# The start of a fused attention and two-layer-pair kernel: another order of its first 24 slots, and low halves of g1 on GpSimd

## The chip, the cores and the metric

The kernel runs on one core of a Trainium2 chip. The core has TensorE (PE in the profile; PEld is its loading of weights), VectorE (DVE), ScalarE (ACT), GpSimd (POOL) and SyncE (SP), which here issues the DMAs. The metric is the device time of one execution in microseconds (us), the median of several runs.

## The reference, cut to what matters

```python
scores = (q @ k.T) / sqrt(64)              # B 4, H 8, S 576, D 64
scores = where((rel >= 0) & (rel < 128), scores - slope[h] * rel, -1e9)
x = softmax(scores) @ v                    # to (2304, 512)
h = x @ w_in                               # 512 -> 2048
P = a0 + a1*h + a2*h**2 + a3*h**3
Q = 1 + |b0|*|h| + |b1|*h**2
y = (P / (Q + 1e-6)) @ w_out               # 2048 -> 512
h = y @ w2_in                              # 512 -> 2048
out = where(h > 0, h, exp(min(h, 0)) - 1) @ w2_out
```

## The kernel before

All products with weights are made of three products in fp16: each operand is scaled by a power of two and split into a high and a low half. The weights are w0 to w3 (`moe_w_in`, `moe_w_out`, and the two of the second pair). A weight comes in eight pieces of 512 KB. Before it can be split, its scale must be known. For this `gram` multiplies each piece with itself into one bank (a "norm product", 8 products of 128x128 each), `column_norms` takes the largest of each row, `top_turn`, `top_across` and `top_over` bring the largest of all to every partition, and `top_scales` makes the scale. The same is done for v, whose first three pieces (n = 0 in `TOPS`) serve the first tiles and whose other nine the later ones. Then ScalarE makes the high half of a piece (`piece_high`) and VectorE the low half (`piece_low`). `TOP_AT`, `GRAM_AT` and `SPLIT_AT` are the slots in which this happens.

The program is one loop over slots s from `FIRST` = -10, written out for every engine in its own order; semaphores join the engines. In slot s:

- Attention works on unit u = s + 10, one pair of heads of one block of 128 queries. TensorE makes the scores (`qk`), VectorE adds the distances (`bias_scores`), ScalarE takes the exponent, VectorE the reciprocals, GpSimd or (from slot 0 to 13) ScalarE normalises, TensorE turns the probabilities (`turn`), ScalarE copies them (`copy_probs`), TensorE multiplies them with v (`pv`), and ScalarE and VectorE write the halves of x (`split_x`, `low_x`). Every fourth slot the next block's queries and keys are turned and copied. In slots -10 to -7 the scores are 128 wide, in slots -6 to -1 they are 256 wide.
- From slot 0 on there is one step of the first pair per slot: `up1` (24 products of 256 columns) for 256 hidden columns of 256 tokens, then `evac1` on ScalarE, `denominator` and `polynomial` on VectorE, `log_exp` on ScalarE, `rational` on VectorE. In the next slot come `high1` on ScalarE and `low1` on VectorE, the two halves of g1, and `down1` takes them two slots after `up1`. Scales and bounds that these steps need come from `factors1(0)` for the first two tiles and `factors1(1)` for the later ones, 17 instructions of VectorE each on numbers of one column, in slots -2 and 7.
- From slot 14 (`LATE`) on there is the second pair too (`up2`, `elu`, `low2`, `down2`). 

SyncE issues the DMAs in a fixed order: queries, keys and v for block 0, v's first pieces, w0 with block 1 in between, then by slot the pieces of w1, the other nine pieces of v, and w2 and w3 as their places come free. The scores go to `score`, one buffer of two halves. Of PSUM's banks `ps_a` and `ps_b` take the scores, `ps_u1` and `ps_u2` the hidden products in turn, and `ps_u2` the norms of w2 and w3. Because of the latter, `up1` stands behind the scores in slots that follow a slot with a norm (3, 5 and 9).

## Time and profile before

| what | value |
|---|---|
| median of 3 runs | 990.9 us (990.37 to 993.07) |
| profiled execution, its own time | 992.75 us |
| profiled execution, span from first to last instruction | 991.0 us |
| TensorE, VectorE, ScalarE, GpSimd busy | 94%, 66%, 61%, 6% of the span |
| bytes moved | 46.72 MB |

A row of a timeline has the start and the length of an instruction, its engine, its line, and what it writes and reads; in brackets stands how long the engine sat idle before it, and what released it. Instructions of one engine can overlap a little; its pace is read from starts. Line L1070 is the bias of the scores, L1168 the denominator, L1107 the low half of a piece, L870 its high half, L509 a norm product, L1196 the low half of g1.

### The profile page before, as it was taken

Reading aid. Unit: us, or ns where it says so; the run is one execution under the profiler, and the core shown is the slowest. Engines: PE = TensorE matmul, PEld = TensorE weight load, DVE = VectorE, ACT = ScalarE, POOL = GpSimd, SP = SyncE. Lnnn points to the kernel's source line nnn. Section 1 sums busy time; section 2 is a strip of 40 time slices with the busy share of each in tenths; the row PEclk is TensorE's granted clock in tenths of the full one; section 3 lists DMA queues with packets and bytes.
Section 4 is the critical chain, followed back from the end, with each engine's and each line's share of the span. In section 5 each row is a group of like instructions: output and inputs, shape, how many; then the busy total and the mean of one; then the engine's idle time right before and its main releaser. Section 6 shows DMA issues by size and latency. Waiting matters only on the chain.

```text
span 991.0 us, 19531 instructions
## 1 busy us (share of the span) xinstructions
PE 934.5 (94%) x7692; PEld 715.1 (72%) x7692; DVE 654.3 (66%) x1430; ACT 601.6 (61%) x1189; POOL 55.4 (6%) x62
## 2 busy tenths in 40 slices
PE   6768889799999999999999999999999999999896
PEld 4557767577777777777777777777777777877563
DVE  4767878988876667666766676666766766663232
ACT  2767768877666666666666666666565655563332
POOL 1200000000000000000000000000000000000000
PEclk9878999899999999999999999999999999999898
DMA  9953431122111101111111111001102000000000
GB/s 269 306 169 117 108 96 33 43 57 65 54 25 33 22 14 23 33 22 15 23 32 23 14 23 34 22 15 25 32 2 36 1 22 1 4 21 2 3 22 21
DMA packets 97178, 46.72 MB, mean 47 GB/s; under 512 B 62336, under 2 KB 93248, under 8 KB 97088
## 3 DMA queue, kind: packets, MB, share of 16 engines
q1 hardware_dynamic: 96800, 45.48, 17.6%
q8 instruction: 61, 1.00, 0.5%
q14 instruction: 29, 0.24, 0.1%
q10 hardware_dynamic: 288, 0.00, 0.0%
HBM read 40.70 MB, written 4.72 MB: 46 GB/s over the span
## 4 chain that ended last, share of the span: by engine, by line
PE 80%; DVE 9%; issue 3%; ACT 3%; DMA 2%; SPq 2%; ACTq 0%; DVEq 0%
PE psum L629 17%; PE psum L631 17%; PE psum L630 17%; PE psum L727 6%; PE psum L728 6%; PE psum L729 6%; PE psum L614 3%; PE psum L567 3%; PE psum L593 2%; DVE w_lo L1107 2%; PE psum L509 1%; DVE temps L1175 1%; DMA y_rows<-small 1%; DMA temps<-moe_w_in 1%; SPq L346 1%
## 5 line engine op out<-in xcount | busy, mean ns | idle before, releaser
L629 PE MATMUL psum<-x_hi,w_hi 128*128 128x256 f16 x576 | 158.6, 275 | 4.5 <-DVE x_lo L1091 4.3
L629 PE MATMUL psum<-g,w_hi 128*128 128x256 f16 x576 | 158.4, 275 | 3.9 <-DVE g L1196 2.9
L630 PE MATMUL psum<-g,w_hi 128*128 128x256 f16 x576 | 158.5, 275 | 0.0
L631 PE MATMUL psum<-g,w_lo 128*128 128x256 f16 x576 | 158.4, 275 | 0.0
L630 PE MATMUL psum<-x_lo,w_hi 128*128 128x256 f16 x576 | 157.9, 274 | 0.0
L631 PE MATMUL psum<-x_hi,w_lo 128*128 128x256 f16 x576 | 157.7, 274 | 0.0
L629 PE MATMUL psum<-late,w_hi 128*128 128x256 f16 x576 | 157.0, 273 | 0.0
L630 PE MATMUL psum<-late,w_hi 128*128 128x256 f16 x576 | 157.0, 273 | 0.0
L631 PE MATMUL psum<-late,w_lo 128*128 128x256 f16 x576 | 157.0, 273 | 0.0
L885 ACT ACTIVATE temps<-psum,small 128x512 f32<-128x512 f32 x72 | 49.3, 685 | 149.6 <-PE psum L631 149.6
L1070 DVE CUSTOM_DVE_ANT_0 score<-psum,rel 128x256 f32<-128x256 f32 (+1 forms) x144 | 51.0, 391 | 98.0 <-PE psum L567 76.0
L727 PE MATMUL psum<-w_hi,late 128*128 128x512 f16 x288 | 110.2, 383 | 5.7 <-DVE late L1205 5.0
L728 PE MATMUL psum<-w_lo,late 128*128 128x512 f16 x288 | 110.2, 383 | 0.0
L729 PE MATMUL psum<-w_hi,late 128*128 128x512 f16 x288 | 110.1, 382 | 0.0
L1200 DVE SCALAR_TENSOR_TENSOR late<-late 128x512 f32<-128x512 f32 x72 | 58.8, 816 | 73.2 <-ACT late L913 73.2
L902 ACT ACTIVATE g<-temps 128x512 f16<-128x512 f32 x72 | 45.4, 630 | 91.7 <-DVE temps L1191 69.0
L483 POOL TENSOR_TENSOR prob<-prob,small 128x512 f32<-128x512 f32 (+1 forms) x58 | 55.2, 952 | 728.1 <-DVE small L1083 728.1
L1168 DVE SCALAR_TENSOR_TENSOR temps<-temps,small 128x512 f32<-128x512 f32 x72 | 54.1, 751 | 61.5 <-ACT temps L886 61.4
L826 ACT ACTIVATE prob<-score,small 128x256 f32<-128x256 f32 (+1 forms) x144 | 68.5, 484 | 17.2 <-DVE small L1070 17.2
L912 ACT ACTIVATE late<-psum,small 128x512 f32<-128x512 f32 x72 | 50.1, 696 | 41.8 <-PE psum L631 41.3
L629 PEld LDWEIGHTS psum<-x_hi,w_hi 128*128 128x128 f16 x576 | 56.6, 98 | 25.3 <-issue 11.9
L629 PEld LDWEIGHTS psum<-g,w_hi 128*128 128x128 f16 x576 | 56.8, 99 | 18.7 <-DVE g L1196 3.3
(139 smaller groups left out, 1840.6 us busy)
## 6 DMA issues: line engine op xcount, KB each, us to landing
late<-moe_w_in SPq DMA_DIRECT2D x13, 512.0 KB, 6.0
v_in<-v SPq DMA_DIRECT2D x19, 256.0 KB, 3.0
q_in<-q SPq DMA_DIRECT2D x16, 256.0 KB, 3.3
k_in<-k SPq DMA_DIRECT2D x16, 256.0 KB, 3.8
out<-final SPq DMA_DIRECT2D x16, 256.0 KB, 2.0
late<-moe_w_out SPq DMA_DIRECT2D x7, 512.0 KB, 4.1
w_hi<-moe_w_out SPq DMA_DIRECT2D x6, 512.0 KB, 6.9
w_lo<-moe_w_out SPq DMA_DIRECT2D x6, 512.0 KB, 6.9
```

Source lines behind the costliest of these rows:

```text
L483: pool.tensor_tensor(unit, unit, recip[:, both].unsqueeze(2).broadcast_to([P, 2, nk]), ALU.mult).then_inc(probs, 1)
L629: pe.matmul(out_ap, ws[0], ms[0], start=first, stop=False, skip_group_check=True)
L630: pe.matmul(out_ap, ws[0], ms[1], start=False, stop=False, skip_group_check=True)
L631: return pe.matmul(out_ap, ws[1], ms[0], start=False, stop=last, skip_group_check=True)
L727: pe.matmul(out_ap, hi, rows[0], start=fb == 0, stop=False)
L728: pe.matmul(out_ap, hi, rows[1], start=False, stop=False)
L729: last = pe.matmul(out_ap, lo, rows[0], start=False, stop=fb == FB - 1)
L826: last = act.activation(prob[:, u % 2, h, 0:nk], score[:, h, 0:nk], ACT.Exp, scale=-1.0, bias=lowest[:, at:at + 1], accum_out=total[:, at: ...
L912: act.activation(e2, ps_u2, ACT.Exp, scale=unscale_h2[u])
L1070: last = dve.tensor_tensor_reduce(out=score[:, h, 0:nk], in0=(ps_a, ps_b)[h][:, 0:nk], in1=far, scale=-slope(2 * p + h), scalar=3e38, op0= ...
L1168: dve.scalar_tensor_tensor(out=d1[n % 2], in0=s1, scalar=abs_b[:, 1:2], in1=d1[n % 2], op0=ALU.mult, op1=ALU.add).then_inc(denom, 1)
L1200: dve.scalar_tensor_tensor(out=r2, in0=e2, scalar=-1.0, in1=r2, op0=ALU.add, op1=ALU.min).then_inc(g2_full, 1)
```

## The change

- The scores of odd units go to a second buffer (`score_too`, in the memory of g1) in slots before 0; there a bias waits only for the exponent two units back.
- On TensorE in those slots `qk` comes first, then the turn, the next block's queries and keys (into other banks), the norm products and the values. The keys are copied before the exponent.
- The norm of v is found in slot -9, that of w0 in -2, that of w1 in 0; `top_over` now spreads 128 values by one product, and VectorE takes their largest in `top_scales`. The two steps `top_turn` and `top_across` go.
- w0 is split in slots -1 to 3 and no longer from -4 on, w1 in slots 1 to 5. Slots 0 to 5 hold eleven pieces, where there were eight.
- The norms of w2 and w3 lie in `ps_a`, so `up1` comes first in every slot. In slots 4 and 8 the scales come at the end of VectorE's slot, and the next `qk` waits for them.
- `low1` of steps 0 to 12 is made by GpSimd in slots 1 to 13.
- `factors1(1)` is gone from slot 7. GpSimd makes most of it in four parts (`other_tiles`) at the ends of slots 3, 5, 6 and 7, and VectorE its reciprocals and one scale (`bound_step`) at the ends of slots 4 to 6.
- SyncE issues block 1 two pieces of w0 earlier, and block 2's queries and keys right after w0; four pieces of w2 go one per slot in slots 0 to 3.

```diff
-ORDER = [(0, n) for n in (0, 5, 6, 7, 1, 2, 3, 4)] + [(1, n) for n in range(8)]
+ORDER = [(0, n) for n in (0, 5, 6, 7, 1, 2, 3)] + [(1, n) for n in range(4)] + [(0, 4)] + [(1, n) for n in range(4, 8)]
...
-SPLIT_AT = (-4, -4, -3, -3, -2, -2, -1, -1) + (0, 0, 1, 1, 2, 3, 4, 5)
+SPLIT_AT = (-1, -1, -1, -1, -1, 0) + (1, 1, 1, 2, 2) + (3, 3, 4, 5, 5)
...
-TOP_AT = (FIRST, -5, -1, 2, 4, 8)
-
-GRAM_AT = ((FIRST,) * 3, (-9, -9, -8, -8, -7, -7, -6, -6), (-4, -4, -3, -3, -3, -2, -2, -2), (0,) * 5 + (1,) * 4,
-           (4,) * 8, (8,) * 8)
-MAGNITUDES, FACTORS = -7, (-2, 7)
+TOP_AT = (-9, -2, 0, 2, 4, 8)
+
+GRAM_AT = ((FIRST, -9, -9), (-7, -7, -6, -5, -4, -3, -3, -2), (0,) * 8, (1,) * 9, (4,) * 8, (8,) * 8)
+MAGNITUDES, FACTORS = -7, -2
+
+BOUND_AT = (4, 5, 6)
...
+        score_too = words(g1_all[:, :, :, :].rearrange("p n h c -> p (n h c)"), 0).rearrange("p (n c) -> p n c", n=4)[:, 0:2]
...
         def q_bank(g):
-            return (ps_b if late_block(g) else ps_o[0]).rearrange("p (n c) -> p n c", n=PAIRS)
+            bank = ps_b if late_block(g) else ps_y[1] if 0 < g and FIRST + 4 * g <= 0 else ps_o[0]
+            return bank.rearrange("p (n c) -> p n c", n=PAIRS)
 
         def k_bank(g):
-            return (ps_a if late_block(g) else ps_b).rearrange("p (n c) -> p n c", n=PAIRS)
+            bank = ps_a if late_block(g) else ps_u1 if 0 < g and FIRST + 4 * g <= 0 else ps_b
+            return bank.rearrange("p (n c) -> p n c", n=PAIRS)
...
-            return (ps_u1, ps_y[0], ps_y[1], ps_y[0], ps_u2, ps_u2)[n][:, 0:P]
+            return (ps_u1, ps_y[0], ps_y[1], ps_y[0], ps_a, ps_a)[n][:, 0:P]
+
+        def top_bank(n):
+            return ps_u2 if TOP_AT[n] < 0 else ps_a
...
+        def score_of(u):
+
+            return score_too if u % 2 and FIRST + u < 0 else score
+
+        def wait_g1(engine, n):
+
+            if n < LATE - 1:
+                engine.wait_ge(g1_early, n + 1)
+            else:
+                engine.wait_ge(g1_ready, n + 2 - LATE)
...
-            for n in range(4):
+            for n in range(2):
                 load_piece(0, n, raw[0, n])
             load_qk(1)
             load_v(1)
-            for n in range(4, 8):
+            for n in range(2, 8):
                 load_piece(0, n, raw[0, n])
             load_v(2)
+            load_qk(2)
...
-                if s == -1:
-                    for n in range(4, 8):
-                        sp.wait_ge(w_lowed, lows_done(0, n - 4))
-                        load_piece(2, n, raw[2, n])
+                if 0 <= s < 4:
+                    sp.wait_ge(w_lowed, lows_done(0, s))
+                    load_piece(2, s + 4, raw[2, s + 4])
...
+            def other_tiles(part):
+
+                hs, turned, line, rest, bound = later[:, 0:2], later[:, 2:4], later[:, 4:5], later[:, 5:6], later[:, 6:7]
+                if part == 0:
+                    pool.wait_ge(x_scaled, 2)
+                    pool.wait_ge(top_done, 4)
+                    chain(pool.tensor_scalar(later[:, 0:1], v_top[:, 1:2], w_top[:, 0:1], 1e18, ALU.mult, ALU.min))
+                    chain(pool.tensor_tensor(later[:, 1:2], later[:, 0:1], later[:, 0:1], ALU.mult))
+                    pool.sem_inc(bound_asked, 1)
+                    pool.tensor_scalar(line, later[:, 0:1], abs_a[:, 3:4], abs_a[:, 2:3], ALU.mult, ALU.add).then_inc(pool_steps, 1)
...
+                    pool.sem_inc(factors, 3)
+
+            def low1(n):
+                pool.wait_ge(g1_high, n + 1)
+                pool.tensor_tensor(g1[n % 2][1], d1[n % 2], g1[n % 2][0], ALU.subtract).then_inc(g1_early, 1)
+
             for s in range(FIRST, FIRST + UNITS):
+                if 1 <= s < LATE:
+                    low1(s - 1)
                 if not scaled_early(s - FIRST):
                     normalise(s - FIRST)
+                if s == BOUND_AT[0] - 1:
+                    other_tiles(0)
+                if s - 1 in BOUND_AT:
+                    other_tiles(BOUND_AT.index(s - 1) + 1)
...
-            def top_turn(n):
+            def top_over(n):
+
                 pe.wait_ge(largest_found, n + 1)
                 if n >= 1:
                     pe.wait_ge(top_done, n)
-                if TOP_AT[n] >= 2:
-                    pe.wait_ge(poly, 2 * TOP_AT[n])
-                pe.transpose(ps_top[0:1, P:2 * P], largest[:, n:n + 1], ident).then_inc(top_turned, 1)
-
-            def top_over(n):
-                pe.wait_ge(top_found, n + 1)
-                pe.matmul(ps_top[:, 2 * P:2 * P + 1], top_low[0:1].broadcast_to([1, P]), ident[0:1, 0:1],
+                if TOP_AT[n] >= 0:
+                    pe.wait_ge(biased, made[0])
+                pe.matmul(top_bank(n)[:, P:2 * P], largest[:, n:n + 1].broadcast_to([P, P]), ident,
                           start=True, stop=True).then_inc(top_spread, 1)
...
+                if FIRST <= u + FIRST - 1 < LATE:
+                    pe.wait_ge(top_done, sum(at < u + FIRST for at in TOP_AT))
...
+                    qk()
                     if u >= 2:
                         turn()
-                    qk()
-                    if s == FIRST:
-                        for n, j in grams_at(s):
-                            gram(n, j)
-                    for n in tops_at(s):
-                        top_turn(n)
+                    next_queries()
+                    prep_keys()
+                    for n, j in grams_at(s):
+                        gram(n, j)
                     if u >= 2:
                         pv()
-                    next_queries()
                     for n in tops_at(s):
                         top_over(n)
-                    prep_keys()
-                    if s > FIRST:
-                        for n, j in grams_at(s):
-                            gram(n, j)
                     if s == -1:
...
-                    for j in range(2) if not tops_at(s - 1) else ():
-                        up1(up, j)
+                    up1(up, 0)
+                    up1(up, 1)
                     pv()
                     qk()
-                    for j in range(2) if tops_at(s - 1) else ():
-                        up1(up, j)
                     next_queries()
+                    down1(down, 0)
                     for n, j in grams_at(s):
                         gram(n, j)
-                    down1(down, 0)
-                    for n in tops_at(s):
-                        top_turn(n)
                     turn()
                     for n in tops_at(s):
-                        top_over(n)
+                        if n < 4:
+                            top_over(n)
                     down1(down, 1)
+                    for n in tops_at(s):
+                        if n >= 4:
+                            top_over(n)
                     prep_keys()
...
+                    if made[0] == 4 * made[3] - 1:
+                        made[3] += 1
+                        copy_keys(made[3] - 1)
...
+                if u > -FIRST:
                     dve.wait_ge(expd, u)
+                elif u >= 2:
+                    dve.wait_ge(expd, u - 1)
...
+                chain(dve.tensor_reduce(norm, top_bank(n)[:, P:2 * P], op=ALU.max, axis=XY.X))
+                if kind == "v" and i:
+                    chain(dve.tensor_tensor(norm, norm, v_norm, ALU.max))
                 elif kind == "v":
-                    chain(dve.tensor_tensor(v_norm, v_norm, found, ALU.max))
-                norm = v_norm if kind == "v" else found
+                    chain(dve.tensor_scalar(v_norm, norm, 1.0, None, ALU.mult))
...
+            def bound_step(n):
+
+                dve.wait_ge(bound_asked, n + 1)
+                if n == 0:
+                    dve.reciprocal(later[:, 2:4], later[:, 0:2]).then_inc(bound_told, 1)
+                elif n == 1:
+                    dve.reciprocal(later[:, 2:4], later[:, 2:4]).then_inc(bound_told, 1)
+                else:
+                    scale_of(later[:, 6:7], g_inv[:, 1:2], g_scale[:, 1:2], bound_told)
...
+            distances()
             copy_queries(0)
-            distances()
...
-                if s == FACTORS[1]:
-                    factors1(1)
-                    for e in range(2):
-                        chain(dve.tensor_scalar(unscale_y[e], w_inv[:, 1:2], g_inv[:, e:e + 1], None, ALU.mult))
...
-                    if s >= 1:
-                        low1(s - 1)
+                    if s >= 0:
+                        for w, n in pieces[:1]:
+                            piece_low(w, n)
                     for n in tops_at(s):
-                        if s >= 0 or s == FIRST:
+                        if n < 4:
                             column_norms(n)
-                    for w, n in pieces[:1]:
-                        piece_low(w, n)
                     if s < 0:
-                        for n in tops_at(s):
-                            top_across(n)
+                        for w, n in pieces[:1]:
+                            piece_low(w, n)
                     if s >= 0:
                         polynomial(s)
+                        reciprocals()
+                        low_x()
                         for n in tops_at(s):
-                            top_across(n)
-                    reciprocals()
-                    if s >= FIRST + 2:
-                        low_x()
-                    if s < 0:
+                            if n >= 4:
+                                column_norms(n)
+                    else:
+                        if s >= FIRST + 3:
+                            low_x()
                         next_queries()
+                        if s > FIRST:
+                            reciprocals()
+                        if s == -1:
+                            reciprocals()
+                            low_x()
                     for n in tops_at(s):
-                        top_scales(n)
+                        if n < 4:
+                            top_scales(n)
                     for w, n in pieces[1:]:
                         piece_low(w, n)
                     if s == MAGNITUDES:
                         magnitudes()
-                    if s == FACTORS[0]:
-                        factors1(0)
+                    if s == FACTORS:
+                        factors1()
                     if s >= 0:
                         rational(s)
+                    for n in tops_at(s):
+                        if n >= 4:
+                            top_scales(n)
+                    if s in BOUND_AT:
+                        bound_step(BOUND_AT.index(s))
```

TensorE in slots -5 and -4, before. L593 is the turn, L567 the scores, L519 and L523 the two steps of the norm, L614 the values, L509 a norm product.

```order
L593 MATMUL psum<-ident,prob 128x128 x2
L567 MATMUL psum<-kT,qT 128x256 x2
L519 MATMUL psum<-ident,small 1x128
L614 MATMUL psum<-probT,v_in 64x128 x2
L523 MATMUL psum<-ident,small 128x1
L593 MATMUL psum<-ident,prob 128x128 x4
L567 MATMUL psum<-kT,qT 128x256 x2
L614 MATMUL psum<-probT,v_in 64x128 x4
```

The same slots now (L663 the turn, L637 the scores, L684 the values, L576 a norm product).

```order
L637 MATMUL psum<-kT,qT 128x256 x2
L663 MATMUL psum<-ident,prob 128x128 x2
L576 MATMUL psum<-late 128x128 x8
L684 MATMUL psum<-probT,v_in 64x128 x2
L637 MATMUL psum<-kT,qT 128x256 x2
L663 MATMUL psum<-ident,prob 128x128 x4
L576 MATMUL psum<-late 128x128 x8
L684 MATMUL psum<-probT,v_in 64x128 x4
```

The scores now stand ahead of the turn, and the norm products of w0, which ended in slot -6 before, lie between the turn and the values.

VectorE from the low half of a piece in slot -1 to slot 0's denominator (L1168), before. L1118 and L1130 to L1134 belong to the norm of w1, L1082 and L1083 are the reciprocals, L1091 the low half of x.

```order
L1082 TENSOR_SCALAR small<-small 128x2
L1083 RECIPROCAL small<-small 128x2
L1091 SCALAR_TENSOR_TENSOR x_lo<-psum,small,x_hi 128x128
L1130 TENSOR_SCALAR small<-psum 128x1
L1133 TENSOR_SCALAR small<-small 128x1
L1134 RECIPROCAL small<-small 128x1
L1107 SCALAR_TENSOR_TENSOR w_lo<-late,small,w_hi 128x1024
L1070 ISA score,small<-psum,rel 128x256
L1070 ISA small 128x1
L1070 ISA score,small<-psum,rel 128x256
L1070 ISA small 128x1
L1168 SCALAR_TENSOR_TENSOR temps<-temps,small 128x512
```

The same place now, from behind the first low half of slot -1 (L1149 and L1150 the reciprocals, L1158 the low half of x, L1174 that of a piece, L1242 the denominator).

```order
L1149 TENSOR_SCALAR small<-small 128x2
L1150 RECIPROCAL small<-small 128x2
L1149 TENSOR_SCALAR small<-small 128x2
L1150 RECIPROCAL small<-small 128x2
L1158 SCALAR_TENSOR_TENSOR x_lo<-psum,small,x_hi 128x128
L1174 SCALAR_TENSOR_TENSOR w_lo<-temps,small,w_hi 128x1024 x3
L1174 SCALAR_TENSOR_TENSOR w_lo<-late,small,w_hi 128x1024
L1137 ISA score,small<-psum,rel 128x256
L1137 ISA small 128x1
L1137 ISA score,small<-psum,rel 128x256
L1137 ISA small 128x1
L1242 SCALAR_TENSOR_TENSOR temps<-temps,small 128x512
```

The norm of w1 has left; two units' reciprocals stand there, and four low halves of w0 in a row lie between the last low half of x and slot 0's bias (L1137).

VectorE in slot 5, from the denominator to the last step of the rational function (L1191), before. L1175 and L1177 are the polynomial.

```order
L1168 SCALAR_TENSOR_TENSOR temps<-temps,small 128x512
L1196 TENSOR_TENSOR g<-temps,g 128x512
L1107 SCALAR_TENSOR_TENSOR w_lo<-w_lo,small,w_hi 128x1024
L1175 TENSOR_TENSOR temps<-temps 128x512
L1177 SCALAR_TENSOR_TENSOR temps<-psum,small,temps 128x512
L1082 TENSOR_SCALAR small<-small 128x2
L1083 RECIPROCAL small<-small 128x2
L1091 SCALAR_TENSOR_TENSOR x_lo<-psum,small,x_hi 128x128
L1184 SCALAR_TENSOR_TENSOR temps<-temps 128x512
L1187 SCALAR_TENSOR_TENSOR temps<-temps 128x512
L1191 SCALAR_TENSOR_TENSOR temps<-temps,small 128x512
```

The same slot now (L1242 the denominator, L1249 and L1251 the polynomial, L1265 the last step, L1236 a step for the later tiles' factors).

```order
L1242 SCALAR_TENSOR_TENSOR temps<-temps,small 128x512
L1174 SCALAR_TENSOR_TENSOR w_lo<-w_lo,small,w_hi 128x1024
L1249 TENSOR_TENSOR temps<-temps 128x512
L1251 SCALAR_TENSOR_TENSOR temps<-psum,small,temps 128x512
L1149 TENSOR_SCALAR small<-small 128x2
L1150 RECIPROCAL small<-small 128x2
L1158 SCALAR_TENSOR_TENSOR x_lo<-psum,small,x_hi 128x128
L1174 SCALAR_TENSOR_TENSOR w_lo<-w_lo,small,w_hi 128x1024
L1258 SCALAR_TENSOR_TENSOR temps<-temps 128x512
L1261 SCALAR_TENSOR_TENSOR temps<-temps 128x512
L1265 SCALAR_TENSOR_TENSOR temps<-temps,small 128x512
L1236 RECIPROCAL small<-small 128x2
```

The low half of g1 is gone from behind the denominator, a second piece is split ahead of the rational function, and a small step closes the slot.

## Rows read from the trace of the kernel before

**Rows 1.** The page: busy time, share and instructions of each engine.
```profile
PE 934.5 (94%) x7692; PEld 715.1 (72%) x7692; DVE 654.3 (66%) x1430; ACT 601.6 (61%) x1189; POOL 55.4 (6%) x62
```

**Rows 2.** Windows by stage: PE, PEld, DVE, ACT, POOL busy, PEclk, DMA share, GB/s.
```profile
0.00:63.79 63.79, 43.23 (x360) 31.84 (x361) 36.34 (x149) 31.03 (x74) 8.91 (x14) 0.89 1.03 289
63.79:201.28 137.49, 115.64 (x1038) 95.23 (x1036) 113.97 (x265) 105.19 (x219) 0.00 (x0) 0.93 0.28 72
201.28:991.00 789.72, 775.65 (x6300) 588.06 (x6298) 503.99 (x1018) 465.39 (x898) 46.54 (x48) 0.99 0.10 23
```

**Rows 3.** Timeline: last norm product of w0, and ScalarE's first piece.
```profile
27.67 0.63 PE L509 MATMUL psum<-temps 128*128 128x128 bf16 x8 [1.10 <-DMA temps<-moe_w_in]
...
32.24 1.15 ACT L870 ACTIVATE w_hi<-late,small 128x1024 f16<-128x1024 f32 x1 [0.88 <-DVE small L1134]
```

**Rows 4.** Windows of slots -6, -4, -2, -1, 0 and 1.
```profile
25.78:29.21 3.43, 2.33 (x27) 1.46 (x23) 1.66 (x9) 1.73 (x6) 1.04 (x1) 1.00 1.10 255
...
32.55:39.93 7.38, 4.96 (x34) 3.69 (x36) 4.36 (x10) 6.38 (x11) 1.12 (x2) 0.54 1.19 266
...
44.54:52.45 7.91, 3.22 (x40) 2.48 (x40) 7.49 (x27) 4.50 (x10) 1.04 (x1) 1.00 1.03 402
52.45:59.30 6.85, 4.81 (x28) 3.05 (x29) 4.41 (x15) 4.01 (x8) 1.04 (x1) 0.57 1.00 245
59.30:70.87 11.57, 9.22 (x94) 7.63 (x93) 7.72 (x16) 8.33 (x16) 0.00 (x0) 0.94 0.34 116
70.87:81.20 10.33, 9.31 (x72) 8.13 (x72) 8.92 (x19) 8.51 (x19) 0.00 (x0) 0.69 0.24 52
```

**Rows 5.** Timeline of TensorE: the first scores.
```profile
9.50 0.80 PE L567 MATMUL psum<-kT,qT 64*128 64x128 f32 x4 [0.78 <-ACT kT L809]
```

**Rows 6.** Timeline: scores, values and turn of a unit, and the copy.
```profile
43.79 0.70 PE L567 MATMUL psum<-kT,qT 64*128 64x256 f32 x4
...
45.18 0.66 PE L614 MATMUL psum<-probT,v_in 128*64 128x128 f32 x8 [0.69 <-ACT probT L845]
...
64.01 0.60 PE L593 MATMUL psum<-ident,prob 128*128 128x128 f32 x4
...
44.55 0.58 ACT L845 ACTIVATE probT<-psum 128x512 f32<-128x512 f32 x1
```

**Rows 7.** Timeline of VectorE: low halves in slot -2 and slot 5.
```profile
47.01 2.03 DVE L1107 SCALAR_TENSOR_TENSOR w_lo<-late,small,w_hi 128x1024 f16<-128x1024 f32 x1
...
116.34 0.69 DVE L1196 TENSOR_TENSOR g<-temps,g 128x512 f16<-128x512 f32 x1 [0.43 <-ACT g L902]
116.95 1.28 DVE L1107 SCALAR_TENSOR_TENSOR w_lo<-w_lo,small,w_hi 128x1024 f16<-128x1024 f32 x1
```

**Rows 8.** GpSimd's normalisation in slot -2; all of L1200, durations min/median/max in ns.
```profile
46.93 1.04 POOL L483 TENSOR_TENSOR prob<-prob,small 128x512 f32<-128x512 f32 x1 [3.56 <-DVE small L1083]
...
L1200 DVE SCALAR_TENSOR_TENSOR late<-late x72: 679/693/1506, 206.2 to 978.0; 128x512 f32<-128x512 f32 x72
```

**Rows 9.** Timeline of VectorE: first and last of the factors in slot 7.
```profile
128.32 0.21 DVE L1147 TENSOR_SCALAR small<-small 128x1 f32<-128x1 f32 x1
...
131.61 0.45 DVE L1259 TENSOR_SCALAR small<-small 128x1 f32<-128x1 f32 x2
```

**Rows 10.** Waits between 59.3 and 199 us: total, times, longest.
```profile
ACT temps L885 <- PE psum L631: 17.2, 6, 3.8
...
DVE g L1196 <- ACT g L902: 3.8, 9, 0.4
```

**Rows 11.** Starts of two successive hidden products; the chain's norm products of w2.
```profile
60.87 0.27 PE L631 MATMUL psum<-x_hi,w_lo 128*128 128x256 f16 x1
60.98 0.27 PE L629 MATMUL psum<-x_hi,w_hi 128*128 128x256 f16 x1
...
101.15 3.79 PE psum L509 x64
```

87 lines of the change are left out of this document (53 added, 34 removed).

## The prediction

> **What bounds the kernel now.** I first read the busy rows and the slices [rows 1], then three windows cut at the first instruction of the rational function in slot 0 and in slot 14 [rows 2]. From 201.28 us on, TensorE is busy 775.65 of 789.72 us: it alone sets the pace, and the change leaves its work there as it is. So a microsecond gained before slot 14 is one gained at the end, and none comes from later. Before that lie two stages. In stage A (0 to 63.79) every engine is idle for a third of the time or more, while the DMA engines are full (share 1.03). In stage B (63.79 to 201.28, fourteen slots, 9.8 us each) TensorE has 115.64, VectorE 113.97 and ScalarE 105.19 us busy in 137.49: no engine is full, they hand one slot's work to each other.
>
> In stage A the reader is to see two things. The last piece of `moe_w_in` is multiplied at 27.67 after waiting for its DMA, and the scale stands at 32.2 [rows 3]; that part is set by DMA, and the change keeps the bytes ahead of that piece. After it the data wait for engines: slot -4 takes 7.38 us and slot -2 7.91 us [rows 4], since eight pieces are split (1.2 us each on VectorE [rows 7], 1.05 on ScalarE [rows 3]), the factors take 3.3 us (the same 17 instructions as from 128.32 to 131.61 [rows 9]), and the scores wait behind all that.
>
> **Stage A, part by part.** (1) The distances move ahead of the first queries. They end at 10.8 now, but the first scores end at 10.3 [rows 5], so 0.5 us is gained. (2) The scores are multiplied before the turn and the norm products, the norm of v moves one slot on, and the exponent of a slot need not be over before the next bias. What then limits a slot of two key blocks goes bias, reciprocal, normalisation on GpSimd, turn, copy, values, next scores: 0.7 + 0.6 + 1.04 + 0.6 + 0.5 + 0.6 + 0.65 plus some 0.3 of hand-over, 5.0 us over two slots (scores, values and copy in [rows 6], GpSimd in [rows 8]), 2.5 each against 3.43 [rows 4]. Short slots I put at 2.1; slots with queries and keys (-7 and -3) at 4.1; slot -9 waits for the norm of v, 3.5. From 10.3 that is 11.8 (-9), 15.3, 17.4, 21.5 (-6), 24.0, 26.6, 29.3 (-3), 33.4 for slot -2. Block 2's queries now come right behind w0, some 0.8 MB more at 289 GB/s [rows 2], by 30: just in time. (3) In slot -2 the norm, its spread by one product instead of two steps, and the scale take 3.5 us, to 36.9; the factors 3.3 more, to 40.5. ScalarE's five pieces run under these (5.2 us, to 42.2), and hide them. (4) In slot -1: bias 0.7, one low half 1.2, ScalarE's copy and exponent to 43.7, reciprocals and the last low x at 44.3. TensorE can start the first hidden product then; at the lower clock, which it has in such gaps (0.54 and 0.57 in [rows 4]), it takes 4 us, and four low halves with one GpSimd normalisation in their way end at 50. Bias 0.7, and slot 0's denominator starts at 51, where it now starts at 63.79. **Gain of stage A: 13 us.** Three of the eight pieces (3.6 us of VectorE) are only postponed; they come back below. Bounds: w0 lands at 28, so a prologue that waited for data alone would bring 4 or 5 us more; if the slots stay at today's 3.4, it brings 5 less. So 8 to 18. The second weight, 11.9 MB in all, needs 41 us at 289 GB/s, and its norm is wanted at 45; v's other pieces, 15.4 MB, need 53, and are wanted at 60. Both are covered, by 4 and 7 us.
>
> **Stage B, part by part.** (5) Thirteen low halves of g1 leave VectorE. Each takes 0.6 us up to the next start [rows 7], and nine of them wait 0.43 us more for ScalarE's high half [rows 10]: 7.8 + 3.8 = 11.6 us. They go to GpSimd, which is idle there, takes 1.04 us for as many elements [rows 8], and is wanted by TensorE only in the next slot: not on the path by itself. But it is in VectorE's way: next to a normalisation that starts 0.1 us before it, a low half of a weight (L1107) takes 2.03 us where another takes 1.28, and L1200 reaches 1.51 with a median of 0.69 [rows 7 and 8]. So each low half costs between 0 and 0.8 us. Nothing in this trace shows GpSimd asking while a two-input VectorE instruction runs, which is what happens here in ten slots (ScalarE's high half ends 0.4 us into the weight's low half, 1.2 us long); in three slots without a piece the psum step, the reciprocals and the low x (1.2 us, unhindered in the trace) hide it. I take 0.5 in ten slots, 5 us. Net 6.6; ends 3.6 and 11.6.
>
> The Trainium skill ("SBUF — State Buffer", Who interferes with whom) says that an instruction of VectorE with two inputs in SBUF and one of GpSimd that reads SBUF exclude each other for their whole length, and that the one issued first decides. The 2.03 us agree. It speaks against this move, and does not say who goes first when one already waits.
>
> (6) The factors of the later tiles, 3.75 us at 128.32 to 132.06 [rows 9], leave VectorE but for five small steps (0.8 us): 3.0. GpSimd's small steps sit between two low halves; `copy_y` of slot 10 is the first that needs them, three slots later. (7) In slots 3, 5 and 9 the hidden product stood behind the scores, since a norm lay in its bank; ScalarE waits 17.2 us for it in six waits between 59.3 and 199 us [rows 10]; the other three belong to slot 0's start (3.5), to the factors of (6) (3.8) and to a short one (0.7), so these three are worth 9.2. That order goes: 9 us. In its place the scores of slots 5 and 9 wait until the scale that is now made last in slots 4 and 8 is there (1.1 us of scale, 0.9 until the new score), some 4 us for both. Net 5. (8) Three more pieces: minus 3.6. (9) What is late next: TensorE. 48 products at 0.11 us, values 0.66, scores 0.70, turn 0.6 [rows 6 and 11] make 7.2 us a slot, 11 with a weight's norm (64 products, 3.79 us). Slots 6 and 7, where VectorE would need 5.2, end at 7.4; that takes back about 2 us. **Gain of stage B: 6.6 + 3.0 + 5 - 3.6 - 2 = 9 us**, with 128.5 us left for fourteen slots, or 9.2 each. TensorE's work in them is 113 us, the bound below which no choice of mine can bring it; VectorE's is 109 plus what GpSimd blocks.
>
> **Sum.** 991.0 - 13 - 9 = 969.0 us of span. The profiled run's own time, 992.75, lies 1.75 over its span and 1.85 over the median of 990.9; so for a median I take 22 off 990.9: 969.
>
> **Rivals.**
> A, the forecast, 958 to 979: chance 0.56.
> B, GpSimd takes back what VectorE gives. It has been asking since the middle of the weight's piece and gets the port as soon as that ends, so the polynomial behind it waits the whole 1.04 us in ten slots, and the small steps hit others. For it: all starts of GpSimd in the trace were followed by a VectorE instruction that waited it out. Stage B then gains 3 to 4 instead of 9, and the small factor steps eat another 1: 975. Chance 0.20. The skill's rule, same page and section, would be this case if a waiting engine comes ahead of the next instruction. Against it: VectorE's next instruction starts 0.08 us before the last ends.
> C, the prologue is better than I have put it: slot -2 starts when w0 lands, at 29, and VectorE keeps the port. 13 + 4.5 + 9 + 4.5: 960 to 956. Chance 0.14.
> D, slower than before: the clock. In slot 1 the granted clock was 0.69, in slots -4 and -1 0.54 and 0.57 [rows 4], each after a stretch in which TensorE had little to do. With a product that starts sooner but waits more often, TensorE could stay at 1.2 GHz for slots 0 to 5. Then a slot is 14.4 us of TensorE where I count on 9.6: 29 us lost against 22 gained, 998. It decides from five slots at the lower level on. Against it: in slot 0 the clock was at 0.94 although slot -1 was at 0.57. Chance 0.03.
> E, the change gives nothing to be measured: the order of issue on SyncE (queries of block 2, which wait for block 1's turn, now stand ahead of the second weight) holds back 4 MB so long that slots 0 and 1 wait some 10 us each for norms: 989. It needs block 1's turn at 30 or later; I have it at 19. Chance 0.04. The remaining 0.03 is for a stall I do not see, either way.
>
> **How the numbers follow.** The likeliest is A with 969. C reaches to 957 and B to about 980, which together hold 9 in 10 before the errors of my slot lengths; I give 957 to 981. Faster by over 0.3% (3 us, about what a measurement of this kernel can tell from none): 0.93; within 0.3%: 0.04; slower: 0.03.
>
> **What would show it.** Slot 0's denominator starts at 47 to 55 and slot 14's at 175 to 184; behind it the distance to the end stays at 789.7 within 1.5 us. Step 2 is right if slots -6 to -4 are 2.3 to 2.8 us long; step 4 if the four low halves run back to back up to slot 0's bias. Step 5 shows as the low half's row on GpSimd at 1.04 us and, in slots 1 to 5, as polynomial rows of 1.2 to 1.7 us (B) or 0.68 (not B). Step 7: ScalarE's wait for the hidden product falls from 17 us to under 6. The prediction is wrong if the part from slot 14 on changes, if the slots stay at 9.8 us, or if TensorE's clock stays at its lower level beyond slot 1.

## The result and the profile after

The changed kernel takes 983.3 us (median of 4 runs, 981.9 to 984.4) where the kernel before takes 990.6 in the same comparison (989.9 to 993.1): a ratio of 0.992, with a 95% interval of 0.990 to 0.993. The profiled execution has a span of 982.6 us. I had forecast 969 and a range of 957 to 981. The direction was right, the size was not: a third of the forecast gain came.

The windows of the changed kernel, cut where [rows 2] are cut, at the first denominator (L1242) of slot 0 and of slot 14. Below them are slots 2, 4 and 13. The columns are those of [rows 2].

```profile
0.00:51.36 51.36, 34.82 (x279) 25.35 (x280) 31.37 (x141) 27.39 (x70) 8.89 (x14) 0.90 1.04 287
51.36:195.39 144.03, 119.44 (x1112) 98.81 (x1110) 118.30 (x248) 109.14 (x223) 27.12 (x28) 0.93 0.35 95
195.39:982.60 787.21, 774.96 (x6302) 587.86 (x6300) 503.90 (x1018) 465.37 (x898) 46.55 (x48) 1.00 0.10 23
71.53:85.85 14.32, 10.36 (x74) 8.00 (x75) 9.74 (x25) 8.83 (x18) 1.91 (x1) 0.77 0.01 2
94.52:111.98 17.46, 13.93 (x131) 12.32 (x132) 9.30 (x24) 8.70 (x18) 1.47 (x1) 0.80 0.53 147
183.65:195.39 11.74, 8.13 (x62) 6.03 (x60) 9.27 (x17) 9.40 (x19) 1.73 (x1) 0.85 0.21 46
```

Stage A took 51.36 us where I said 51, and gained 12.4. Stage B was to shrink from 137.49 to 128.5 and grew to 144.03: minus 6.5 instead of plus 9. The rest took 787.21 instead of 789.72. That is no gain of the change, as twelve more kernels show below: from the fifteenth denominator to the last both profiles take 686.3 us, and the 2.5 lie behind the last one (103.4 against 100.9), where TensorE's granted clock was 0.94 before and 0.97 after. 12.4 - 6.5 + 2.5 is the 8.4 us between the spans.

The lengths of the slots, from one denominator's start to the next (each is the difference of two starts; "before" is the profile of the rows above):

| slot | 0 | 1 | 2 | 3 | 4 | 5 | 6 | 7 | 8 | 9 | 10 | 11 | 12 | 13 | sum |
|---|---|---|---|---|---|---|---|---|---|---|---|---|---|---|---|
| before | 9.7 | 8.4 | 12.9 | 7.9 | 12.5 | 7.4 | 9.9 | 8.9 | 11.8 | 9.6 | 8.4 | 8.9 | 10.8 | 10.5 | 137.5 |
| after | 10.2 | 9.9 | **14.3** | 8.7 | **17.5** | 8.5 | 6.6 | 7.8 | 10.9 | 9.3 | 8.7 | 8.7 | 11.0 | 11.7 | 144.0 |

Two slots stand out. In slot 4 TensorE and VectorE wait for data. The rows are TensorE's norm products of w2, VectorE's largest values of them (L1181), and what SyncE issues ten microseconds before (SPq is its DMA queue; L363 loads a block of q, k or v, L411 a piece of a weight).

```profile
99.58 1.03 PE L576 MATMUL psum<-late 128*128 128x128 bf16 x8 [3.30 <-DMA late<-moe_w_in]
...
104.07 0.29 DVE L1181 TENSOR_REDUCE small<-psum 128x1 f32<-128x128 f32 x1 [4.79 <-PE psum L576]
...
84.51 0.37 SPq L363 DMA_DIRECT2D v_in<-v  x1
84.92 0.58 SPq L411 DMA_DIRECT2D late<-moe_w_in  x1
85.55 1.05 SPq L411 DMA_DIRECT2D w_hi<-moe_w_in  x2
86.64 1.79 SPq L411 DMA_DIRECT2D w_lo<-moe_w_in  x2
88.48 2.81 SPq L411 DMA_DIRECT2D late<-moe_w_in  x1
```

Six of w2's eight pieces (6, 0 to 3 and 7) are issued behind `load_v(4)`, which waits until the values of a unit in slot 3 are multiplied, at 84.5. The last piece is issued at 88.5; the norm products stand still for it for 3.3 us, until 99.6, and VectorE 4.8 us. The granted clock of the slot is 0.80, so the products behind the wait run in part at the lower level.

In slot 2 TensorE stands still twice, before the first product of `down1` (L699) and inside its second half, before the last six products:

```profile
73.77 0.37 PE L699 MATMUL psum<-g,w_hi 128*128 128x256 f16 x1 [4.89 <-issue]
...
80.43 0.28 PE L699 MATMUL psum<-g,w_hi 128*128 128x256 f16 x1 [1.72 <-DVE w_lo L1174]
...
73.39 0.28 DVE L1181 TENSOR_REDUCE small<-psum 128x1 f32<-128x128 f32 x1
```

The first wait is marked "issue"; VectorE's rows show what it is for. v's norm was multiplied into the bank into which `down1` writes, and its largest values (L1181) are found at 73.39, behind the denominator and a low half of slot 2. The second wait is for the low half of piece (1,3).

And in twelve of the thirteen slots with a low half on GpSimd (L547) one instruction of VectorE takes 0.8 to 1.0 us longer: the polynomial in slots 1, 2, 6, 11 and 13, the weight's low half in slots 3, 4, 9, 10 and 12, the denominator in slots 5 and 7. Slot 1, after, and below it slot 10:

```profile
62.82 1.74 POOL L547 TENSOR_TENSOR g<-temps,g 128x512 f16<-128x512 f32 x1 [16.75 <-ACT g L964]
...
62.26 1.28 DVE L1174 SCALAR_TENSOR_TENSOR w_lo<-late,small,w_hi 128x1024 f16<-128x1024 f32 x1
63.46 1.65 DVE L1249 TENSOR_TENSOR temps<-temps 128x512 f32<-128x512 f32 x1
...
155.60 1.33 POOL L547 TENSOR_TENSOR g<-temps,g 128x512 f16<-128x512 f32 x1 [7.99 <-ACT g L964]
...
155.17 0.75 DVE L1242 SCALAR_TENSOR_TENSOR temps<-temps,small 128x512 f32<-128x512 f32 x1
155.84 2.18 DVE L1174 SCALAR_TENSOR_TENSOR w_lo<-w_hi,small 128x1024 f16<-128x1024 f32 x1
```

GpSimd starts at 62.82 while VectorE is in a low half of w1 (L1174) with 0.7 us to go, and ends 1.74 us later, 1.0 after the end of that low half. The polynomial behind it (L1249, 0.68 us alone) takes 1.65: it waited for the whole of GpSimd's work, about 1.0 us. In slot 10 GpSimd starts while VectorE is in the denominator, and the low half behind that takes 2.18 instead of 1.28. This is the mechanism of my rival B, though only five of the instructions held back are polynomials. The Trainium skill ("SBUF — State Buffer", Who interferes with whom) says that a VectorE instruction with two inputs in SBUF and a GpSimd instruction that reads SBUF exclude each other, and that the one issued first keeps the other out to its end. The rows agree with the exclusion; in them GpSimd, already waiting, goes ahead of VectorE's next instruction.

### The profile page after: what moved, and what is told of

Read it like the earlier page. It is cut to its first block, busy times and chain, and to the rows that moved or that the text cites. A ratio compares the mean times of both kernels' runs of the same rounds, so it can differ in the third digit from the quotient of the medians.

```text
span 982.6 us, 19544 instructions
## 1 busy us (share of the span) xinstructions
PE 929.2 (95%) x7686; PEld 712.0 (72%) x7686; DVE 653.6 (67%) x1403; ACT 601.9 (61%) x1189; POOL 82.6 (8%) x90
## 4 chain that ended last, share of the span: by engine, by line
PE 82%; DVE 9%; issue 3%; DMA 3%; ACT 2%; POOL 0%; SPq 0%; DVEq 0%; ACTq 0%
PE psum L699 17%; PE psum L700 17%; PE psum L701 17%; PE psum L795 6%; PE psum L796 6%; PE psum L797 6%; PE psum L684 3%; PE psum L637 3%; PE psum L663 3%; DVE w_lo L1174 2%; PE psum L576 2%; DVE temps L1249 1%; DVE temps L1242 1%; DMA late<-moe_w_in 1%; DMA y_rows<-small 1%
## 5 line engine op out<-in xcount | busy, mean ns | idle before, releaser
L699 PE MATMUL psum<-g,w_hi 128*128 128x256 f16 x576 | 158.6, 275 | 7.6 <-issue 4.9
L699 PE MATMUL psum<-x_hi,w_hi 128*128 128x256 f16 x576 | 158.5, 275 | 3.1 <-DVE x_lo L1158 2.5
L699 PE MATMUL psum<-late,w_hi 128*128 128x256 f16 x576 | 157.1, 273 | 0.0
L1137 DVE CUSTOM_DVE_ANT_0 score<-psum,rel 128x256 f32<-128x256 f32 (+1 forms) x134 | 47.6, 393 | 101.5 <-PE psum L637 81.4
L509 POOL TENSOR_TENSOR prob<-prob,small 128x512 f32<-128x512 f32 (+1 forms) x58 | 55.3, 953 | 581.7 <-DVE small L1150 581.7
L964 ACT ACTIVATE g<-temps 128x512 f16<-128x512 f32 x72 | 45.3, 630 | 92.3 <-DVE temps L1265 69.3
L1242 DVE SCALAR_TENSOR_TENSOR temps<-temps,small 128x512 f32<-128x512 f32 x72 | 55.9, 776 | 57.3 <-ACT temps L948 57.2
L699 PEld LDWEIGHTS psum<-g,w_hi 128*128 128x128 f16 x576 | 56.9, 99 | 23.1 <-issue 7.9
L699 PEld LDWEIGHTS psum<-x_hi,w_hi 128*128 128x128 f16 x576 | 56.6, 98 | 22.9 <-issue 11.6
L700 PEld LDWEIGHTS psum<-g,w_hi 128*128 128x128 f16 x576 | 56.9, 99 | 13.3
```

Of the source, the lines that this page charges most:

```text
L509: pool.tensor_tensor(unit, unit, recip[:, both].unsqueeze(2).broadcast_to([P, 2, nk]), ALU.mult).then_inc(probs, 1)
L699: pe.matmul(out_ap, ws[0], ms[0], start=first, stop=False, skip_group_check=True)
L700: pe.matmul(out_ap, ws[0], ms[1], start=False, stop=False, skip_group_check=True)
L1137: last = dve.tensor_tensor_reduce(out=score_of(u)[:, h, 0:nk], in0=(ps_a, ps_b)[h][:, 0:nk], in1=far, scale=-slope(2 * p + h), scalar=3e38 ...
L1242: dve.scalar_tensor_tensor(out=d1[n % 2], in0=s1, scalar=abs_b[:, 1:2], in1=d1[n % 2], op0=ALU.mult, op1=ALU.add).then_inc(denom, 1)
```

## The experiments

Each kernel was timed in three rounds beside the kernel before. "First" is the start of the first denominator, "B" the stretch from there to the fifteenth, "rest" what is behind it.

| kernel | time, us | ratio (95%) | first | B | rest |
|---|---|---|---|---|---|
| after | 983.3 | 0.992 (0.990 to 0.993) | 51.4 | 144.0 | 787.2 |
| e1: v's block 4 behind w2 | 979.8 | 0.989 (0.988 to 0.991) | 54.3 | 137.5 | 786.9 |
| e2: low half on VectorE | 984.5 | 0.994 (0.991 to 0.996) | 54.9 | 144.3 | 785.8 |
| e3: GpSimd's low half later | 977.7 | 0.987 (0.986 to 0.989) | 52.2 | 137.0 | 786.2 |
| e4: before, low half on GpSimd | 990.8 | 0.999 (0.998 to 1.001) | 64.6 | 134.5 | 787.1 |
| e5: v's norm earlier | 983.9 | 0.992 (0.990 to 0.995) | 53.2 | 144.6 | 787.6 |
| e6: one score buffer | 983.5 | 0.992 (0.989 to 0.994) | 53.2 | 141.9 | 786.1 |
| e7: e1 and e3 | 973.6 | 0.982 (0.979 to 0.985) | 54.1 | 134.3 | 787.6 |
| e8: e1, e3, e5 and e9 | 971.0 | 0.979 (0.977 to 0.981) | 53.2 | 129.7 | 787.4 |
| e9: both pieces first in slot 2 | 982.1 | 0.991 (0.989 to 0.993) | 52.9 | 140.7 | 787.5 |
| e10: e8, low half on VectorE | 975.0 | 0.984 (0.982 to 0.985) | 52.3 | 133.5 | 787.2 |
| e11: e8, keys first in slot 13 | 969.7 | 0.978 (0.976 to 0.981) | 54.3 | 128.1 | 787.0 |
| e12: e8, factors on VectorE | 974.4 | 0.983 (0.982 to 0.985) | 53.1 | 132.9 | 787.4 |

The rest is 785.8 to 787.6 us in all thirteen, e4 among them, whose code from slot 14 on is that of the kernel before. With the place of the 2.5 us, behind the last denominator at a lower clock, I take the 789.72 of [rows 2] as that execution's own; the change gives nothing there. Each stretch in the table is read from one execution, and the time is a median, so the stretches don't add up to it exactly.

### e1: the data of slot 4

```diff
-                    if g <= FULL and FIRST + 4 * g - 4 == s:
+                    if g <= FULL and g != 4 and FIRST + 4 * g - 4 == s:
                         load_v(g)
...
+                if s == 3:
+                    load_v(4)
                 if s == TOP_AT[4]:
```

> The changed kernel with one move on SyncE: the load of block 4's v, which waits for the values of unit 11 (slot 3), goes behind the pieces of w2 instead of standing ahead of five of them. Theory (queue): slot 4's norm products waited 3.3 us for the last piece of w2 and then ran at the lower clock, because the pieces were issued only from 84.5 us on. Then the pieces are issued by 72 us, slot 4 (denominator 4 to 5) falls from 17.5 to 12 to 13 us, and the time by 4 to 5.5 us against the changed kernel, to 978 to 979. Rival (late anyway): slot 4 is long because its norm products, its scale and the next scores stand in a row; the DMA wait is only part of it. Then slot 4 stays at 15 or more and the time falls by less than 2 us.

Slot 4 takes 11.22 us where it took 17.46; every other slot up to 12 is as before this edit, to 0.03 us. The window of slot 4 in e1, and its norm products, now in a row:

```profile
97.51:108.73 11.22, 10.99 (x131) 9.81 (x132) 9.11 (x25) 8.71 (x18) 1.46 (x2) 1.00 0.57 156
...
97.74 2.00 PE L578 MATMUL psum<-late 128*128 128x128 bf16 x32 [0.49 <-DVE small L1139]
99.57 1.08 PE L578 MATMUL psum<-w_hi 128*128 128x128 bf16 x16
100.49 1.08 PE L578 MATMUL psum<-w_lo 128*128 128x128 bf16 x16
...
74.87 1.69 SPq L411 DMA_DIRECT2D late<-moe_w_in  x1
```

The last piece is now issued at 74.9. The 6.2 us were one wait on SyncE, with w2 queued behind it: 3.3 us of standing still, and the rest goes with the clock, 0.80 then and 1.00 now. The time falls by 3.5 us and not by 6, less than I had expected, because the price varies: the six profiles that have this queue (after, e2, e3, e5, e6, e9) show slot 4 at 17.5, 15.9, 15.0, 15.4, 15.2 and 13.2 us, so 4 us above 11.2 is the usual one. The dearest has the longest wait for the piece (3.3 us) and the lowest granted clock (0.80), the cheapest the shortest (1.8 us) and 1.00. Between the two profiles the spans differ by 3.9 us, since e1's first denominator came 3 us later than after's, which is not the edit's (last section).

### e2, e3, e4 and e10: the low half on GpSimd

e2 gives it back to VectorE, behind the denominator. e3 leaves it on GpSimd but lets it start only when the step's first polynomial instruction is over:

```diff
             def low1(n):
                 pool.wait_ge(g1_high, n + 1)
+                pool.wait_ge(poly, 2 * n + 3)
                 pool.tensor_tensor(g1[n % 2][1], d1[n % 2], g1[n % 2][0], ALU.subtract).then_inc(g1_early, 1)
```

> The changed kernel with the low halves of g1 of slots 1 to 13 back on VectorE, behind the denominator. Theory (port): beside GpSimd's low half an instruction of VectorE with two inputs in SBUF takes 0.9 to 1.0 us longer in every slot, and that is as much as the low half costs on VectorE itself (0.6, with 0.43 of waiting 1.0). Then the part from the first to the fifteenth denominator stays at 144 us within 2, and the time at 981 to 985. Rival (the move pays): it is 6 to 11 us longer, 989 to 994, since 13 instructions and nine waits come back.

> The changed kernel; GpSimd's low half waits in addition for the first step of that slot's polynomial, so that it runs beside the second step (one input in PSUM), the reciprocals and the low half of x (1.2 us in all). Theory (port): VectorE's polynomial and weight rows fall back to 0.68 and 1.28 us, GpSimd's row to 1.04 to 1.2, and the part from the first to the fifteenth denominator falls by 6 to 11 us (VectorE is on the chain in most slots, in slots 2, 4 and 8 TensorE is): 973 to 978. Rival (no port): the later low half makes nothing shorter; the part stays at 144 or grows by up to 2 us.

> The kernel before with one part of the change alone: the low halves of g1 of slots 1 to 13 on GpSimd. Theory (port): what VectorE saves it loses to the port; 989 to 992, within 2 us of the kernel before. Rival (the move pays, and the change lost it elsewhere): 6 to 11 us faster, 980 to 985.

In e2 stage B is as long as after, 144.25 for 144.03. Slot 2 is 2.6 us longer, since v's norm now waits for a low half more; slots 3, 5 to 7, 9, 10 and 12 are 0.2 to 0.4 shorter, slot 4 with its wait for data 1.6, slots 1 and 11 0.2 longer, slot 13 1.0. As it stands in the change, the move to GpSimd is worth nothing.

e3 gains 7.1 us in stage B. The groups of VectorE show where, between 51 and 196 us: first after, then e3 (line, shapes, count, busy us, mean ns of one, idle before).

```profile
L1249 DVE TENSOR_TENSOR temps<-temps 128x512 f32<-128x512 f32 x14 | 14.2, 1011 | 0.0
L1242 DVE SCALAR_TENSOR_TENSOR temps<-temps,small 128x512 f32<-128x512 f32 x15 | 13.1, 872 | 4.1 <-ACT temps L948 4.1
L1174 DVE SCALAR_TENSOR_TENSOR w_lo<-w_hi,small 128x1024 f16<-128x1024 f32 x8 | 11.9, 1504 | 0.2 <-DVE small L1199 0.2
```

```profile
L1250 DVE TENSOR_TENSOR temps<-temps 128x512 f32<-128x512 f32 x15 | 10.3, 684 | 0.0
L1243 DVE SCALAR_TENSOR_TENSOR temps<-temps,small 128x512 f32<-128x512 f32 x15 | 11.2, 748 | 4.2 <-ACT temps L949 4.2
L1175 DVE SCALAR_TENSOR_TENSOR w_lo<-w_hi,small 128x1024 f16<-128x1024 f32 x8 | 10.1, 1279 | 0.2 <-DVE small L1200 0.2
L1150 DVE TENSOR_SCALAR small<-small 128x2 f32<-128x2 f32 x15 | 8.5, 567 | 0.0
```

The polynomial is back at its 684 ns, the denominator at 748, the low halves at 1279. But the exclusion has not gone, it has moved to a cheaper place: slot 1 in e3,

```profile
63.91 0.68 DVE L1250 TENSOR_TENSOR temps<-temps 128x512 f32<-128x512 f32 x1
64.62 0.75 DVE L1252 SCALAR_TENSOR_TENSOR temps<-psum,small,temps 128x512 f32<-128x512 f32 x1
65.29 0.63 DVE L1150 TENSOR_SCALAR small<-small 128x2 f32<-128x2 f32 x1
...
64.74 1.16 POOL L548 TENSOR_TENSOR g<-temps,g 128x512 f16<-128x512 f32 x1 [17.84 <-DVE temps L1250]
```

GpSimd starts 0.12 us into the instruction that reads PSUM (L1252), which is not lengthened (0.75), and holds only the small step behind it: 0.63 us for an instruction on two columns that takes 0.16 in a free slot. So the slot loses 0.45 us instead of 0.9.

What the placement alone is worth shows where slot 4 has its data, in e7 against e1: 0.2 to 0.5 us in each of nine slots, 3.9 together, less 0.6 in slot 13, so 3.2 in the stretch. Of e3's 7.1 us another 2.5 lie in slot 4 (the wait for data, which varies), and 0.7 in slots 0 and 13.

e4 asks the same of the kernel before: stage B 3.0 us shorter than in [rows 2], the time not to be told from the old one (0.998 to 1.001). Its profile is of one of its fastest executions (988.0 us, of 987.7 to 992.3), so the 3.0 are not its usual gain.

e10 puts the low half back on VectorE in the repaired kernel e8.

> The kernel of three edits with the low half of g1 back on VectorE, behind the denominator, as in the kernel before. It shows what the move to GpSimd is worth once data and norm no longer cover it and once GpSimd waits its turn. Theory V (a low half on VectorE costs its 0.6 us and a wait of 0.4 for the high half, as my step 5 counted, and in the kernel of three edits nothing takes it back): ten slots 0.6 to 1.0 us longer, the stretch from the first to the fifteenth denominator 136 to 140 us where the kernel of three edits has 129.67, the time 977 to 981. Rival X (ScalarE or TensorE limits these slots as well): 1 to 3 us longer in all, the time 972 to 974.

The stretch grows by 3.9 us and the time by 4.0, between the two expectations. So a well placed low half on GpSimd is worth 3.9 us. The bad placement costs 3.2 of them, which leaves 0.6 (without slot 13, whose length goes with the clock, 3.2 and 3.9, or -0.7). So the move as the change has it is worth nothing that can be told from zero, as e2 says directly. My step 5 had 6.6.

### e5, e8 and e9: slot 2

e5 moves v's norm to the end of slot 1:

```diff
                     for n in tops_at(s):
-                        if n < 4:
+                        if n < 3:
                             column_norms(n)
...
                         reciprocals()
                         low_x()
+                        if s == TOP_AT[3] - 1:
+                            column_norms(3)
```

> The changed kernel with one edit: VectorE finds the largest values of v's norm (column_norms(3)) at the end of slot 1, where the norm products are ready, and no longer in slot 2 behind its denominator and a low half. Theory N (that step holds down1 of slot 2 and with it the turn): TensorE's 4.89 us idle in slot 2 shrinks below 2 us, slot 2 takes 11 to 12 us where it takes 14.32, the stretch from the first to the fifteenth denominator 141 to 142 us where it takes 144.03, and the time falls by 2 to 3 us to about 981. Rival M (the low half of piece (1,3), which VectorE makes only after slot 2's polynomial, holds the second half of the hidden product anyway): slot 2 stays within 1 us of 14.3, the time within 1 us of 983.

My theory fell, the rival held: slot 2 stays at 14.31 us. TensorE in slot 2 of e5:

```profile
70.72 0.28 PE L699 MATMUL psum<-g,w_hi 128*128 128x256 f16 x1
...
75.62 0.28 PE L699 MATMUL psum<-g,w_hi 128*128 128x256 f16 x1 [1.31 <-DVE w_lo L1174]
...
80.97 0.40 PE L699 MATMUL psum<-g,w_hi 128*128 128x256 f16 x1 [4.52 <-DVE w_lo L1174]
```

The wait for the norm is gone: the first half of `down1` now runs right behind the scores, from 70.72. Its second half waits 1.31 us for the low half of piece (1,2), and then 4.52 us, where it was 1.72, for that of piece (1,3), which stands on VectorE behind the polynomial, the reciprocals and the whole scale of v. So the one wait hid the other. e9 moves only that piece forward (`pieces[:2]` instead of `pieces[:1]` ahead of the polynomial in slot 2):

> The changed kernel with one edit: in slot 2 VectorE makes both low halves, (1,2) and (1,3), ahead of its polynomial. v's norm is still found in slot 2, now behind them. With that norm alone moved, slot 2 had stayed at 14.31 us; with both edits it took 9.52. Theory P (either wait alone is enough to hold TensorE: the norm holds the first half of down1, the piece (1,3) the second): the norm is found 1.2 us later than in the changed kernel, the second wait is gone, slot 2 takes 12.5 to 14 us, and the time falls by less than 2 us, to 981.5 to 983.5. Rival Q (the place of the pieces is the whole cause): slot 2 at 9.5 to 10.5 us, the time 979.

As expected, slot 2 takes 13.75 us: v's norm is now found at 77.07, 2.1 us later in the slot than after (I had said 1.2; the rest is GpSimd's, which goes ahead of the second piece), and TensorE waits 6.99 us for it.

```profile
77.07 0.28 DVE L1181 TENSOR_REDUCE small<-psum 128x1 f32<-128x128 f32 x1
...
77.45 0.37 PE L699 MATMUL psum<-g,w_hi 128*128 128x256 f16 x1 [6.99 <-issue]
```
e8 has both edits, and those of e1 and e3:

> The changed kernel with all three edits (v's block 4 behind w2's pieces; GpSimd's low half held until the first polynomial instruction has ended; v's norm found at the end of slot 1), and both low halves of slot 2 ahead of its polynomial. Theory: slot 2 at 11 to 12 us and slot 4 at about 11; the stretch from the first to the fifteenth denominator takes 128 to 130 us, as I had forecast for the change itself (128.5), and the time is 970 to 973. Rival: slot 2's gain is lost in slot 3, where the weight's low halves are late, and the time is that of the two edits alone.

Slot 2 takes 9.52 us, 4.8 less than after, where the edits alone brought 0.0 and 0.6. (Some 0.9 of it is GpSimd's, whose low half no longer stretches the two of VectorE: 3.38 us in e9, 2.47 in e8.) The two waits in the second half of `down1`, for pieces (1,2) and (1,3), in e8:

```profile
75.11 0.28 PE L702 MATMUL psum<-g,w_hi 128*128 128x256 f16 x1 [1.31 <-DVE w_lo L1177]
...
76.30 0.28 PE L702 MATMUL psum<-g,w_hi 128*128 128x256 f16 x1 [0.37 <-DVE w_lo L1177]
```

Against e7, which differs by these two edits alone, slot 2 is 4.8 us shorter too (14.32 there), and the median time 2.7. Slot 3 doesn't give it back (8.26, as in e3). e8 takes 971.0 us, 2% less than before and 1.3% less than the change as it was. It is the better kernel by every one of its runs (970.3 to 972.1 against 981.9 to 984.4).

### e7: do they add up?

> The changed kernel with two edits: v's block 4 issued behind the pieces of w2, and GpSimd's low half held until the step's first polynomial instruction has ended. Alone they took 6.5 us and 7.1 us off the stretch between the first and the fifteenth denominator (144.03). Theory: they act in different places but for slot 4 (6.2 us from the first, 2.5 from the second), so the stretch takes 131 to 133 us, and the time is 973 to 976. Rival: once one is gone, TensorE's own work or the hand-over sets the slots, and the two together bring 8 to 9 us, the stretch 135 to 136, the time 977 to 978.

Slot 4 is at 11.22 and slots 1 to 12 otherwise are e3's. The stretch is 134.25 us, 1.3 above the upper end of what I expected (slots 0 and 13 are 0.4 and 0.6 longer than in e3), the time 973.6, as expected (its four runs spread from 971.7 to 977.8, and the profile is of the longest).

### e6: the second score buffer

```diff
-            return score_too if u % 2 and FIRST + u < 0 else score
+            return score
...
-                if u > -FIRST:
+                if u >= 1:
                     dve.wait_ge(expd, u)
-                elif u >= 2:
-                    dve.wait_ge(expd, u - 1)
```

> The changed kernel with the second score buffer undone: in slots before 0 every bias writes to the same buffer again and waits for the exponent of the unit before. Theory S (as my step 2 had it, the two buffers are what takes a slot of two key blocks from 3.4 to 2.3 us): slots -6 to -4 take 2.9 to 3.4 us each, the first denominator comes 2 to 4 us later than 51.4, at 54 to 56, and the time rises by as much, to 985 to 987. Rival T (the scores ahead of the turn do it alone, and the exponent is over by then in any case): slots and time stay as they are, within 1 us. Rival W (w0's landing sets the scale anyway): the slots grow but the first denominator does not move.

The buffer does nothing. The biases of slots -6, -5, -4 and -3 start at 24.08, 26.39, 28.69 and 31.55 in e6 and at 24.11, 26.41, 28.72 and 31.58 in e5, which has two buffers. So the exponent of the unit before is not what a bias waits for there, and the 2.3 us of a slot come from the rest of the new order. That it is the scores ahead of the turn is likely, but no run put them back.

### e11: the keys in slot 13

In the windows above slot 13 is 1.3 us longer than before. TensorE waits there for the copied keys, 3.61 us after and 3.11 in e8 where it was 0.96 in the kernel before, and in e8 it then runs at its lower level for 5 us (products 0.21 us apart instead of 0.11, granted clock 0.72 over the slot). e11 copies the keys ahead of ScalarE's normalisation in that slot.

> The kernel of three edits with a fourth: in slot 13 ScalarE copies the keys of the next block ahead of its normalisation and no longer behind it. In slot 13 TensorE sits idle 3.1 us for that copy before the values, and then runs at 1.2 GHz for 5 us. Theory K: the values start about 1.4 us sooner, slot 13 takes 10 to 10.8 us where it takes 12.05, the time 969 to 970. Rival L (the normalisation is then late for the turn, or the clock falls all the same): slot 13 within 0.5 us of 12.05, the time 970.5 to 971.5.

The wait falls from 3.11 to 2.24 us and slot 13 from 12.05 to 10.55. In the time the two kernels overlap (969.7 of 967.5 to 971.4, against 971.0), so a gain of 1 us is not shown. Nor is the slot's length a proof: with no edit there it was 9.8 to 12.7 us in the other kernels, with waits of 0.6 to 3.7 us and granted clocks of 0.72 to 0.89. Why the wait is longer than before no run shows.

### e12: the factors of the later tiles

> The kernel of three edits with the factors of the later tiles back on VectorE, 19 small instructions ahead of slot 7's bias, as in the kernel before; GpSimd's four parts and VectorE's three small steps go. Theory F (my step 6: they cost VectorE 3.75 us there and cost GpSimd nothing): slot 7 takes 10.5 to 11.2 us where it takes 7.39, slots 4 to 6 get 0.2 to 0.8 us shorter in all, and the time rises by 2.5 to 3.5 us to about 974. Rival G (TensorE is at the limit in slot 8 and waits less there, or slots 4 to 6 give back what their small steps took): less than 1 us.

The time rises by 3.5 us, as expected, but not by what I said. The 19 instructions hold back slot 7's bias by 3.0 us, and slot 7 itself then is 2.5 us longer (9.88 for 7.39). TensorE in e12:

```profile
122.58 0.37 PE L698 MATMUL psum<-x_hi,w_hi 128*128 128x256 f16 x1 [4.49 <-DVE x_lo L1157]
122.74 0.42 PE L699 MATMUL psum<-x_lo,w_hi 128*128 128x256 f16 x1
122.95 0.42 PE L700 MATMUL psum<-x_hi,w_lo 128*128 128x256 f16 x1
...
119.31:129.19 9.88, 6.61 (x38) 4.51 (x38) 5.54 (x15) 4.64 (x13) 1.16 (x1) 0.65 0.58 147
```

After 4.49 us without work its products start 0.21 us apart, twice the 0.11 of [rows 11], and the granted clock of the window is 0.65. So 24 products cost 2.5 us more. Slot 13 gives 2.2 back: the lower level lies ahead of its wait for the keys in this profile and not behind it, so TensorE arrives later, waits 1.09 us instead of 3.11 and multiplies the values in 0.66 us instead of 1.12.

## Why the prediction was wrong, step by step

**What bounds the kernel.** Right: the rest behind slot 14 stayed as it was, and what was lost and won before it came out at the end. The 789.7 that I took for it was 2.5 us too much for a usual execution. That did not spoil the forecast, since I subtracted gains only.

**Stage A, steps 1 to 4.** Right to about a microsecond in the one profile: biases at 11.96, 16.09, 18.36, 22.55, 24.86, 27.16, 30.03 and 33.88, where I had 11.8, 15.3, 17.4, 21.5, 24.0, 26.6, 29.3 and 33.4; first denominator at 51.36 for 51. Over the twelve profiles with this start it lies at 51.4 to 54.9, in the middle at 53.2, and the two with the old start are at 63.8 and 64.6. So the usual gain is 11 us where I had 13, inside my 8 to 18. The cause within step 2 was half wrong: the second buffer does nothing (e6), and the new order does it all. In slots -1 and 0 step 4 came as I said: four low halves from 45.3 to the bias at 50.7.

**Step 5, the low half on GpSimd: the first term that failed.** Forecast 6.6 net, measured 0.6 (3.9 from e8 against e10, less 3.2 from e1 against e7). I had both rows for it, 2.03 for 1.28 and 1.51 for 0.69 [rows 7, 8], and named the case in which GpSimd gets the port as rival B with a chance of 0.20. (That every start of GpSimd in the trace was followed by a VectorE instruction that waited it out, as I wrote there, was not so: the steps behind the one at 54.97 were not held.) I took 0.5 us of the 1.04 in ten slots on the ground that VectorE's next instruction starts 0.08 us before the last one ends. The runs show that this does not help it: a GpSimd instruction that already waits goes first. After, it cost VectorE 0.8 to 1.0 us in each of twelve slots, some 11 us in all (polynomial 1011 for 684 ns, denominator 872 for 748, and the low halves), which is as much as the 11.6 that I had taken off.

**Step 6, the factors: right** in its direct cost, 3.0 forecast and 3.0 at slot 7's bias (e12). That the totals agree as well, 3.2 in stage B and 3.5 in time, is partly luck: the clock in slot 7 adds 2.5, which I had no term for, and slot 13 takes 2.2 back.

**Step 7: the second that failed, by what it left out.** I looked at slots 3, 5 and 9, where the order scores before `up1` had cost time. ScalarE's wait for the hidden product fell as I said in kind, not in size:

(the wait between 50 and 195 us: total, times, longest)

```profile
ACT temps L947 <- PE psum L701: 10.5, 5, 3.1
```

17.2 us in six waits before, 10.5 in five now, where I had "under 6". Of the norm of v I had only said that it moves. The product that writes its bank, the step on VectorE that frees it and the piece that follows were never put in a row for slot 2. That is 4.8 us (e8 against after). Once it was repaired the step's own gain was there: the slots ahead of the three, 2, 4 and 8, took 37.2 us together before, 42.7 after and 31.7 in e8, 5.5 less than before, where I had 5 net; the other terms of these slots are in that number.

**Steps 8 and 9.** The three more pieces were not measured singly. With the data in time slot 4 takes 11.22 us and slot 8 10.94, where I had 11 for a slot with a weight's norm, TensorE being busy for 10.99 of the 11.22.

**What I had no term for: SyncE, 6.2 us.** I had rival E, in which the new order of issue holds back data, put it at slots 0 and 1, priced it at the whole gain and gave it 0.04. The mechanism was there at another place. Pieces 4 to 7 of w2 used to be issued in slot -1; now they go one per slot, and pieces 6 and 7 stand behind `load_v(4)` with the first four. I had checked w1 and v against the data rate, and not w2, and no load against the wait ahead of it.

**The sum.** From the forecast 128.5 us of stage B: 6.0 for the low half, 6.2 for the data, 4.8 for slot 2, less 1.5 which the other terms together came out better: 144.0. In e8, with the causes repaired, the stretch is 129.7: of the 15.5 us that stage B missed, 14.4 came back by moving one load, one wait of GpSimd, one norm and one piece. The 1.5 is what is left over, not a measured gain. The range ended at 981, below the time, since it summed errors of terms I had and left no room for a slot that no term looked at. B and E were treated as alternatives with the other one absent; both held at once.

## What to carry over

When earlier stages get shorter, walk every wait of the DMA queue again with the new times, piece by piece for each weight: a load that waits for an engine holds back all that is queued behind it. A step that frees a bank must stand in a row with the product that writes it next; where two waits end close together, moving either alone shows nothing (0.0 and 0.6 us here), both together 4.8. And work moved from VectorE to GpSimd cost VectorE 0.9 us a slot here where it started beside instructions with two SBUF inputs, and 0.45 beside one that reads PSUM and ahead of small ones: tie its start to such a place.

## What the runs showed of the hardware

- A GpSimd instruction (128x512, two inputs) that begins while VectorE runs one with two SBUF inputs takes up to 1.91 us (1.74 in slot 1) instead of 1.04 to 1.16 and then delays VectorE's next by 0.8 to 1.0. Against VectorE's instruction with one input in PSUM it costs neither anything, but a two-column step behind it takes 0.63 us instead of 0.16. Steps on one column are not held: in the kernel before, GpSimd's normalisation runs from 54.97 to 56.01, and the one-column steps at 55.47 (L1133) and 55.66 (L1134) take 0.15 and 0.17 us, as they do elsewhere; e4 shows the same (0.15 at 55.98, inside 55.48 to 56.52).
- TensorE's clock has a start of its own. The products of the scores in slot -8 take, after and in e1:

```profile
15.56 0.49 PE L637 MATMUL psum<-kT,qT 64*128 64x128 f32 x4 [1.38 <-DVEq L1204]
...
16.02 0.80 PE L639 MATMUL psum<-kT,qT 64*128 64x128 f32 x4 [1.38 <-DVEq L1206]
```

The same four products took 0.80 us in slots -10 and -9 of each profile that I read there (after, e1, e3, e5, e8, e10, e11). After and in e3 TensorE had its upper level (2.4 GHz) from 13.7 us on, with a fall back between 17 and 20; in the other five it kept to the lower one (1.2 GHz) until 21 to 24, although the granted clock of the windows says 1.00 there: it is the durations that have to be read. This goes with first denominators at 51.4 and 52.2 against 52.3 to 54.3. In the five further profiles with this start (e2, e6, e7, e9, e12) the scores of slot -8 take 0.80 us too, and the first denominators lie at 52.9 to 54.9. How much of that is the clock's is not shown: the first scores themselves start anywhere from 9.5 to 11.1. The Trainium skill ("TensorE: Matmul & The Clock Gate", Part 1: The HAM clock gate) says that the same kernel gets its first rise sooner or later from run to run; these profiles agree, with 13.7 to 24 us. No run here tried to bring it forward.
- The level also fell within stage B after TensorE had stood still for 3 to 5 us (slots 2 and 4 after: 4.9 and 3.3 us, granted clock 0.77 and 0.80; slot 7 in e12: 4.5 us, 0.65). In e12 that cost 2.5 us besides the 4.5. After 2.5 us it fell in some executions and not in others: slot 7 took 7.8 us after, at 1.00, and 9.4 in e5 and 9.5 in e9, with the same wait, at 0.82.
